# A drain on GpSimd, and the rounding of the second expert weights moved, in a fused attention and mixture-of-experts kernel

## The reference

```python
# 1. attention, 4 x 8 heads, 576 rows of 64: softmax over the 32 largest scores of a row
# 2. h = maximum(maximum(x @ w1, x @ w2), x @ w3); x = h @ w_out      2304 tokens, 512 -> 768 -> 512
# 3. experts, E = 8, D = 512, F = 1024:
logits = x @ w_gate + modality_bias[modality_id]
e_idx = np.argmax(logits, axis=1)
...
gate_w = probs[np.arange(N), e_idx]
for e in range(E):
    mask = e_idx == e
    if not mask.any():
        continue
    h = np.maximum(x[mask] @ w1[e], 0.0)
    out[mask] = gate_w[mask, None] * (h @ w2[e])
```

## Time and profile before

| | us |
| --- | --- |
| median of 3 runs | 984.05 |
| lowest and highest | 980.38, 984.11 |
| the profiled execution, its own time | 973.69 |
| its span, first to last instruction | 972.1 |
| mean granted TensorE clock in it | 0.991 |
| TensorE busy | 915.5 (94%) |
| VectorE busy | 716.3 (74%) |
| GpSimd busy | 657.5 (68%) |
| ScalarE busy | 580.5 (60%) |

### The profile page before, as it was taken

How to read it: one execution, slowest core, us unless ns; L and a number is a source line. 1 busy time by engine, 2 the same in 40 slices (tenths; PEclk the granted TensorE clock), 3 DMA queues, 4 the chain that set the end, 5 groups by cost and what they waited for, 6 DMA issues and landing times.

```text
span 972.1 us, 18042 instructions
## 1 busy us (share of the span) xinstructions
PE 915.5 (94%) x5324; PEld 678.7 (70%) x5325; DVE 716.3 (74%) x2191; ACT 580.5 (60%) x1226; POOL 657.5 (68%) x623
## 2 busy tenths in 40 slices
PE   4698788999999999999999999999999999989995
PEld 1255567677676667677676677675876998888894
DVE  5999999999999999999999999995305421331210
ACT  2577777877787787778787687775324122332211
POOL 7999988988888897988888887965252321221221
PEclk9999999999999999999999999999999999999998
DMA  6722211312122221222221122111051160133110
GB/s 208 241 58 57 58 47 41 117 46 70 52 58 62 52 64 57 58 57 59 62 58 57 42 69 63 36 36 36 12 189 54 49 224 33 49 135 119 43 54 32
DMA packets 61591, 70.85 MB, mean 73 GB/s; under 512 B 7776, under 2 KB 42880, under 8 KB 61504
## 3 DMA queue, kind: packets, MB, share of 16 engines
q1 hardware_dynamic: 57584, 59.43, 20.2%
q0 software_dynamic: 3920, 10.40, 3.4%
HBM read 59.05 MB, written 10.76 MB: 72 GB/s over the span
## 4 chain that ended last, share of the span: by engine, by line
PE 82%; issue 7%; DVE 5%; ACT 1%; POOL 1%; ACTq 0%; DVEq 0%; POOLq 0%
PE m_ps L1371 18%; PE m_ps L1448 10%; PE m_ps L1392 10%; PE s_ps L1314 9%; PE t_ps L1328 8%; PE s_ps L1431 8%; PE o_ps L1344 7%; PE m_ps L1385 6%; DVE top L1119 3%; PE o_ps L1431 2%; PE m_ps L1399 1%; DVE upper L1121 1%; PE t_ps L1420 1%; DVE work L1121 1%; PE m_ps L1396 1%
## 5 line engine op out<-in xcount | busy, mean ns | idle before, releaser
L776 POOL TENSOR_TENSOR scores<-scores,below 128x576 f32<-128x576 f32 x144 | 200.7, 1423 | 67.9 <-ACT below L906 67.3
L1371 PE MATMUL m_ps<-xT,w_sb 128*128 128x192 f32 x1152 | 200.7, 329 | 1.2 <-ACT xT L950 1.2
L1371 PEld LDWEIGHTS m_ps<-xT,w_sb 128*128 128x128 f32 x1152 | 188.1, 192 | 2.3 <-ACT xT L950 1.5
L1119 DVE MAX8 top<-upper 128x8 f32<-128x288 f32 x384 | 159.3, 447 | 0.4 <-issue 0.3
L1121 DVE MATCH_REPLACE8 upper<-top,upper 128x288 f32<-128x288 f32 x288 | 125.3, 442 | 0.2 <-issue 0.2
L914 ACT ACTIVATE probs<-scores,shift 128x576 f32<-128x576 f32 x144 | 111.4, 783 | 15.5 <-issue 15.5
L1328 PEld LDWEIGHTS t_ps<-ident,probs 128*128 128x128 f32 x720 | 80.9, 142 | 56.0 <-issue 50.1
L943 ACT COPY probsT<-t_ps 128x640 f32<-128x640 f32 x192 | 103.2, 563 | 25.5 <-PE t_ps L1328 22.2
L784 POOL TENSOR_SCALAR probs<-probs,inverse 128x576 f32<-128x576 f32 x144 | 106.0, 765 | 15.9 <-DVE inverse L1103 15.9
L1328 PE MATMUL t_ps<-ident,probs 128*128 128x128 f32 x720 | 108.9, 283 | 6.6 <-ACT probsT L943 6.6
L1314 PE MATMUL s_ps<-k_sb,q_sb 64*64 64x288 f32 (+1 forms) x576 | 100.1, 454 | 15.3 <-ACT fall L931 6.1
(11 more groups left out here) (203 smaller groups left out, 1721.9 us busy)
## 6 DMA issues: line engine op xcount, KB each, us to landing
k_sb<-keys_t SPq DMA_DIRECT2D x48, 288.0 KB, 3.0
v_sb<-values SPq DMA_DIRECT2D x48, 256.0 KB, 2.7
raw<-e_w SPq DMA_DIRECT2D x12, 1024.0 KB, 5.1
q_sb<-queries_t SPq DMA_DIRECT2D x48, 96.0 KB, 1.9
maxout_rows<-x_rows SPq DMA_DIRECT2D x18, 256.0 KB, 2.0
w_sb<-w SPq DMA_DIRECT2D x2, 1536.0 KB, 10.4
v_sb<-values SPq DMA_DIRECT2D x48, 32.0 KB, 2.6
stage<-w_t SPq DMA_DIRECT2D x1, 1536.0 KB, 7.8
```

What stands on the lines that cost most here:

```text
L776: nc.gpsimd.tensor_tensor(scores[:, r % RING, i, :], scores[:, r % RING, i, :], below[:, i, :], ALU.subtract).then_inc(masked_ready, 1)
L1119: nc.vector.max(best, src).then_inc(topk_step, 1)
L1371: ins = nc.tensor.matmul(dst[:, a * BLK:(a + 1) * BLK], w_sb[:, w, c, (first + a) * P:(first + a + 1) * P], xT[:, m % 2, c, b % SPAN * BLK ...
```

## The change

On GpSimd a drain is placed between fetch and scatter, in chunk 0 and in each turn of its loop. On ScalarE and on VectorE the block that splits the two halves of w2 ahead of an expert's first chunk is taken out. Instead, inside the loop over chunks, behind the part of product tile 0, the first half (piece 2) is split, and behind that of tile 3 the second half (piece 3), if this is the expert's first chunk (c < 1) and the expert isn't the star (a > 0). The tests stand in the loop body and so are made in each chunk.

```diff
--- before.py
+++ after.py
@@ -90,6 +90,7 @@
 PIECES = 4
 PIECE = 2 * D * F2 // P // PIECES
 H_BANKS = 3
+PIECE_AT = {0: 2, 3: 3}
 FIRST_TURNS = ((), (0, 1), ())
 FIRST_MIDDLE = 2
 COUNT_LATE_AT = 2
@@ -870,6 +871,7 @@
             for i in range(XT):
                 pool.wait_ge(x2_stored[i], 16 * SUPERS)
             fetch(1, second)
+            pool.drain()
             store_rows(0)
             pool.wait_ge(tables_ready, 1)
             n_chunks = pool.value_load(totals_i[0:1, 1:2], min_val=2, max_val=NCH)
@@ -1070,13 +1073,15 @@
             n_used = act.value_load(totals_i[0:1, 0:1], min_val=1, max_val=E)
             with act.Fori(0, n_used) as a:
                 chunks, first = used_expert(act, a)
-                with act.If(a > 0):
-                    for n in range(PIECES // 2, PIECES):
-                        high_piece(a, n)
                 with act.Fori(0, chunks) as c:
                     g = act.snap(first + c)
                     for f in range(FB2):
                         h_high_part(g, f)
+                        if f in PIECE_AT:
+
+                            with act.If(c < 1):
+                                with act.If(a > 0):
+                                    high_piece(a, PIECE_AT[f])
                     for n in range(SUBS):
                         out_rows(g, n)
                         for m in TURNS[n]:
@@ -1275,13 +1280,15 @@
             n_used = dve.value_load(totals_i[0:1, 0:1], min_val=1, max_val=E)
             with dve.Fori(0, n_used) as a:
                 chunks, first = used_expert(dve, a)
-                with dve.If(a > 0):
-                    for n in range(PIECES // 2, PIECES):
-                        low_piece(a, n)
                 with dve.Fori(0, chunks) as c:
                     g = dve.snap(first + c)
                     for f in range(FB2):
                         h_low_part(g, f)
+                        if f in PIECE_AT:
+
+                            with dve.If(c < 1):
+                                with dve.If(a > 0):
+                                    low_piece(a, PIECE_AT[f])
                     for n in range(SUBS):
                         x_low_part(g + 1, TURNS[n])
                         if n == 0:
```

## The result

| | us |
| --- | --- |
| the changed kernel, median of 5 runs | 971.73 (970.05 to 972.48) |
| the kernel before beside it, median of 5 | 982.05 (980.38 to 984.11) |
| ratio, 95% interval | 0.9895 (0.9874 to 0.9916) |
| the profiled execution after, its span | 970.9 |

The change won 1.05%, 10.3 us, where 4.3 were forecast. The kernel is still bound by TensorE. First the chunk with the stop. Busy time by stretches of the changed kernel: the chunk before it, chunk 3, the chunk behind it (columns as in the earlier trace rows).

The account below looks back on a forecast made before the run. The prediction took the kernel to be bound by TensorE's matmuls (82% of the chain); 2.49 us of waiting and 1.83 of slow clock gave -4.31, all other terms 0: 984.05 - 4.31 = 979.7 us (-0.44%), range 976.5 to 984.3.

Parts of the forecast that it names:

- the stop: Chunk 3, ahead of TensorE's fourth product tile: 2.49 us of waiting for the first hTl, forecast to vanish.
- The halves of w2: Second expert's first chunk (chunk 3): splitting them behind tiles 0 and 3 makes nothing late, 34.78 - 39.09 = -4.31 us.
- The 1.0 us reserves: Chunk 3: hTl 1 and hTl 4 ready 1.0 us before TensorE wants them for tiles 4 and 7.
- The clock: Chunk 3, two tiles behind the wait: TensorE's slow clock costs 1.83 us and goes once the wait goes.
- a small miss costs only itself: Chunk 3: a short TensorE wait would not lower its clock, as 0.80 us idle between 740 and 760 did not.
- a clock that falls all the same: Rival, chunk 3: clock falls for a cause other than the wait; only 2.49 us won, 981.6 us; chance 5%.
- GpSimd beside the pieces: Chunk 3: gathers slowed by VectorE's remainders, second landing by 872.3 with 3 us to spare; taken as 0.
- The tests: Looped chunks, ScalarE and VectorE behind tiles 0 and 3: 0.1 to 0.3 us a place, covered; taken as 0.
- The drain: GpSimd, between the next chunk's gathers and the wait for scaled rows: both ends 0 for the time; taken as 0.
- Some 2.4 us late in chunk 0: Upper end for the drain: if it lasted until gathers landed, chunk 0's first scatter is this late; no engine waits.
- The level: Whole kernel: the timed median of 984.05 us lies 10.4 above the profiled execution, a difference carried over unchanged.

Follow-up runs that it names:

- the change run again: The changed kernel itself, timed once more beside the kernel before on the chip of a later set of runs: 972.56 us against 980.46, ratio 0.9906.
- the run of pieces only: The change without its drains, only the halves of w2 moved behind tiles 0 and 3, against the kernel before: 969.80 us against 974.50, ratio 0.9952.

## Why the prediction was wrong

- **The halves of w2: right.** The term of -4.31 us is 4.34 in the profile, and -4.7 in time by itself. The 1.0 us reserves held: hTl 1 was done at 868.32, 1.1 us ahead of tile 4. ScalarE entered its loop at 862.8, in time to take up tile 0 at 863.25.
- **The clock: right about this stop, too simple in general.** The fall went with the stop of 2.49 us, and a stop of 1.13 us left the clock alone. But the prediction also said that a small miss costs only itself, by the earlier trace rows. TensorE has two idle times, of 0.38 and 0.33 us, ahead of chunk 0, the same in every profile. In that of both pieces behind tile 0 they were followed by a fall, as in that of the change run again, above:

```profile
744.00:748.00 4.00, 3.29 (x25) 3.08 (x24) 1.38 (x2) 1.99 (x5) 0.00 (x0) 0.87 0.17 66
748.00:750.00 2.00, 2.00 (x8) 2.00 (x8) 1.18 (x7) 0.17 (x1) 0.00 (x0) 0.50 0.00 0
```

  The first three product tiles of chunk 0 took 8.94 us there (6.86 and 2.08) and 6.52 in the run of pieces only, 2.4 us lost. In the other ten profiles the clock stayed at 1.00 in that place. So the length of idle time alone doesn't decide, and what does stays open. The prediction's rival of a clock that falls all the same had such a fall in mind for chunk 3, where none came.
- **GpSimd beside the pieces: right, and hidden.** The first gather in chunk 3 took 2.33 us in place of 1.06 and the info copy 1.58 in place of 0.88; nobody waited.
- **The tests: right, 0.**
- **The drain: wrong, and this is the failed step.** The prediction put its lower end at 0: "it is no gain, since what ends that idle time is ScalarE's rows, and nothing that the drain could tidy up is late". That looks at what waits behind the drain in the loop, and there it is true (the drain in chunk 0 made one scatter late, and nobody waited for it). It doesn't look at the other end: the program closes with a drain on GpSimd anyway, and what a drain has to clear adds up from one drain to the next. From the last scatter at 963.23 to 972.1 there are 8.9 us, and 2.7 for the scatter to land leaves 6 that no term of the prediction looks at. The row was in the trace of before (L402, 5303 ns at 966.6). No view of waits has it, and the chain of waits ends with that last scatter, at 964.2 in a span of 972.1; only a look at the end of the span by line shows it. With 61 of the 64 software DMAs cleared ahead of the last drain, at 82 ns each, the term is -5.0 us, and the sum -9.3: 984.05 less 9.3 is 974.7, and the ratio 0.9905, in the measured interval.
- **The page that was weighed.** The Trainium skill (PSUM — Partial Sum Buffer, Engine vs sequencer instructions) says that a drain waits for its engine to go fully idle. Taken as the end of the last gather's issue, as the prediction took it, this is too short here: the drain at 941.7 outlasted that issue, which ended at 944.5, by 2.8 us, until the rows had landed, and at the end of the program, with GpSimd idle and all rows landed, a drain still took 5.30 us. The measurement decides.
- **The bounds of the drain.** "Some 2.4 us late in chunk 0" was right in kind: the scatter at 783.39 has 4.86 us of issue ahead of it. In the run with one drain in the last turn it starts at 780.61, 2.8 us earlier, and nothing behind it came sooner for that (209.30 us from chunk 0's first product to the last y_sb there, 209.36 here).
- **The level.** I carried over 10.4 us from the profiled execution to the median and said nothing of where they come from. The stop of ScalarE goes with 5 to 8 us of such a difference (5.22 in the unchanged kernel run again, 8.14 in the changed one). The profiled execution of before did not have it; that its timed runs did is read from their level alone and not shown. It cost nothing in the ratio, but a forecast in us holds only as far as that level does.

No experiment gave a version faster than the change.

## What to carry to other kernels

Read the span to its last microsecond, and compare its end with that of the chain of waits: what lies between the last useful instruction and the end is made of instructions too, and the drain of the engine that issues software DMAs was 5 us of 972. Its length goes by what has been issued since the last drain, so one drain late in the program, under idle time of that engine, takes it off the end. Work that an expert's start needs only in its second stage can stand behind tiles of the first, if the layout by old durations leaves about 1 us at each tile that waits for it.

## What the runs showed of the hardware

- A drain on GpSimd took 42 ns and 82.2 ns for each software DMA issued since the last drain (289 ns for 3, 622 for 7, 2445 for 29, 3167 for 38, 5303 for 64), and while DMAs were on their way it lasted until they had landed, 5.6 to 8.4 us in the changed kernel. With 61 issued and the last three on their way it took 7.87 us and ended 2.6 us behind their landing, not 5.0: the two overlap.
- The same two idle times of TensorE, 0.38 and 0.33 us, were followed by a granted clock of 0.50 in two profiled executions and of 1.00 in ten.
- ScalarE stood for 4 to 9 us in all on something that no record of the profile shows, between 714 and 725 us whatever the kernel, in some sets of runs and not in others.
